# Lead-in of a fused attention and mixture kernel: keys and queries with neighbouring tokens in a partition, block means of the values as matrix products, loads in another order

## The chip, the core and the metric

The kernel runs on one NeuronCore of a Trainium2 chip. The core has TensorE for matrix products (it reads the on-chip memory SBUF and writes the accumulator memory PSUM, eight banks of 512 fp32 words in each of 128 partitions), VectorE and ScalarE for work on elements (both read and write PSUM and SBUF), GpSimd for constants, conversions and some DMA issues, and the sync engine SP, which issues most of the DMAs. Each engine works through its own queue of instructions in order; they meet in semaphores. A wait holds up everything behind it in that engine's queue. DMAs run on 16 DMA engines shared by all queues. The metric is the time of one execution on the device in microseconds (us).

## What is computed

Three stages follow each other. This case is about the first one only, and about its first half (the first of two batches).

```python
# q, k, v: (2, 8, 768, 64) fp32; block = 32, window = 16
k_sum = k.reshape(B, H, nb, block, D).max(axis=3)
v_sum = v.reshape(B, H, nb, block, D).mean(axis=3)      # 24 block means for each head
scores_l = scale * np.matmul(q, k.transpose(0, 1, 3, 2))
scores_s = scale * np.einsum('bhsd,bhnd->bhsn', q, k_sum) + np.log(block)
# scores_l outside |i - j| < 16 masked; softmax over both; then
out = np.matmul(a, np.concatenate([v, v_sum], axis=2))
# stage 2: dense mixture, sum over 4 experts of p_e * relu(x @ w1[e]) @ w2[e], x (1536, 512)
# stage 3: mixture of 8 experts with a skip score, one expert for each computed token
```

## The kernel before

**Tasks.** Attention is cut into 16 tasks `a`: two batches, two halves `s` of 384 queries, four pairs `n` of heads (`PAIRS`). One pair of heads fills 128 partitions (2 x 64). The keys of a pair are prepared once, for both halves of the batch: tasks 0 to 3 ("wide", `LEAD` = 4) prepare the keys of pairs 0 to 3. A task has six units of 64 queries; each unit sees a window of 96 keys and the 24 block maxima, `KW` = 120 columns.

**The path of a task.** SP loads keys (`load_keys`, L442) and queries (`load_queries`, L449) with tokens in partitions, one token of 64 numbers (256 bytes) in each run. TensorE transposes them into PSUM (`transpose_keys` L1750, six transposes of 128x128; `transpose_queries` L1760, three). ScalarE copies the windows of the keys (`copy_keys`, L850 to L852) and the queries (`copy_queries`, L858) to SBUF; VectorE takes the block maxima (`keys`, L1111 to L1116). TensorE forms the scores (`qk`, L1771, 24 products on tiles of 64x64). VectorE adds the mask and takes the negated maximum (`mask`, L1124, six), ScalarE takes exponentials in place (`exps`, L864, six), VectorE normalises (`norm`, L1132 to L1136, two). TensorE transposes the weights (`turn(a, h)`, L1785, three for each of two halves h), ScalarE evacuates them (`evac_t`, L870), TensorE multiplies with the values (`pv`, L1799, 24 products), ScalarE and VectorE split the result into a high and a low part (`high_o` L875, `low_o` L1142).

**Block means.** `v_all` holds for each unit 96 rows of values (`load_windows`) and 24 rows of block means. VectorE makes the means: `sum_values(c)` takes the values of four heads, 96 partitions with one block of 32 tokens each, halves them five times by additions (L1154: 1024, 512, 256, 128 and 64 columns) and scales (L1156). There are four such calls; c = 0 and 1 (first batch) stand on VectorE's queue ahead of `lead(0)` and `lead(1)`. GpSimd then spreads the means by DMA inside SBUF (`first_sums`, L732), two transfers for each task.

**Order in the lead-in.** It is written out by hand for each engine. On TensorE: keys, queries and scores of task 0, keys and queries of pair 1, and then `lead(a)` for a = 0, 1, 2: `spare` (14, 12 and 12 transposes of the identity, L1888, whose result nobody reads), `turn(a, 0)`, `qk(a + 1)`, `transpose_keys(a + 2)` while there are any, `transpose_queries(a + 2)`, `pv(a - 1)`, `turn(a, 1)`. Then `turn(3, 0)`, `pv(2)`, `turn(3, 1)`, `qk(4)`, `pv(3)`. From there on the first layer of stage 2 fills TensorE between the pieces of attention (L1845 to L1851 for the first block of features, then L1737 to L1739). In a lead ScalarE's order is `exps(a, 1)`, `copy_keys(a + 2)`, `copy_queries(a + 2)`, `exps(a + 1, 0)`, `evac_t(a, 0)`, `high_o(a - 1)`, `evac_t(a, 1)`; VectorE's is `mask(a + 1, 0)`, `norm(a, 1)`, `mask(a + 1, 1)`, `keys(a + 2)`, `norm(a + 1, 0)`, `low_o(a - 1)`. After the leads VectorE forms the low parts of the first layer's weights (`low_w1`, L1191, four pieces) with `low_o(2)` and `low_o(3)` between them. Their high parts are cast by GpSimd (`high_w1`, L737) from loads that GpSimd issues itself (`first_w1`, L723).

PSUM in the lead-in: banks 0 and 1 take transposed keys, 2 queries, 4 and 5 scores, 6 and 3 the two halves of `turn`, 7 the result of `pv`.

## Time and profile before

| | us |
|---|---|
| median of 3 runs | 728.18 |
| lowest, highest | 726.92, 729.25 |
| the profiled execution | 728.09 |
| its span, first to last instruction | 726.4 |

The profile shows one execution. Engines: PE is TensorE's products, PEld its loading of stationary operands, DVE is VectorE, ACT ScalarE, POOL GpSimd, SPq the queue of SP. A busy time of a group of pipelined instructions reaches to the end of the last one, so the next may start before it. The granted clock of TensorE (PEclk) is given as a share of 2.4 GHz; 0.5 is 1.2 GHz. Busy shares by engine over the span: PE 97%, PEld 80%, DVE 56%, ACT 39%, POOL 9%.

### The profile page before, as it was taken

How to read it: one execution, taken by the hardware profiler on the slowest of the kernel's cores; microseconds unless marked ns; L12 is line 12 of the kernel's file. 1: busy time of each engine (PE TensorE's matmuls, PEld its weight loads, DVE VectorE, ACT ScalarE, POOL GpSimd, SP SyncE). 2: the span in 40 equal slices, each digit the busy share in tenths (PEclk: the TensorE clock that was granted, in tenths of full speed). 3: DMA queues.
4: the chain of work that ended last, by engine and by line, in shares of the span. 5: the costliest groups of instructions: out<-in, count | busy, mean ns of one | idle time of the engine just before them, and what ended most of it. 6: DMA issues, size and time to landing. Idle time of an engine off the chain costs nothing.

```text
span 726.4 us, 12344 instructions
## 1 busy us (share of the span) xinstructions
PE 703.5 (97%) x4499; PEld 580.5 (80%) x4500; DVE 403.6 (56%) x1042; ACT 281.5 (39%) x653; POOL 66.2 (9%) x97
## 2 busy tenths in 40 slices
PE   5699999999999999999999999999999999999997
PEld 4588898898989889988988998899899884444444
DVE  4887674552895684754756364466447217453441
ACT  4745454451345534631621451064036112552430
POOL 2612000000000000000000000100000003232221
PEclk9989999999999999999999999999999999999999
DMA  9995632120709717713976739124530996799800
GB/s 205 216 209 107 134 82 64 32 48 12 279 17 335 322 51 291 284 63 103 418 301 278 261 116 363 53 107 179 226 116 3 373 361 232 288 394 393 332 2 22
DMA packets 92384, 139.36 MB, mean 192 GB/s; under 512 B 55172, under 2 KB 55456, under 8 KB 90656
## 3 DMA queue, kind: packets, MB, share of 16 engines
q1 hardware_dynamic: 89664, 133.89, 53.4%
q0 software_dynamic: 2656, 4.66, 2.0%
q8 instruction: 35, 0.57, 0.3%
q14 instruction: 29, 0.24, 0.1%
HBM read 104.05 MB, written 34.98 MB: 191 GB/s over the span
## 4 chain that ended last, share of the span: by engine, by line
PE 92%; DVE 5%; ACT 1%; issue 1%; DMA 0%; POOL 0%; SPq 0%; POOLq 0%; DVEq 0%; ACTq 0%
PE ps L1737 15%; PE ps L1739 15%; PE ps L1738 15%; PE ps L1987 8%; PE ps L1989 8%; PE ps L1988 8%; PE ps L2126 7%; PE ps L2098 7%; PE ps L1799 2%; PE ps L1771 2%; PE ps L1785 1%; PE ps L1930 1%; PE ps L2111 1%; PE ps L1750 1%; DVE acc L1154 1%
## 5 line engine op out<-in xcount | busy, mean ns | idle before, releaser
L1987 PE MATMUL ps<-xt_hi,wb_hi 128*128 128x384 f32 x336 | 112.8, 336 | 0.0
L1989 PE MATMUL ps<-xt_hi,wb_lo 128*128 128x384 f32 x336 | 112.4, 334 | 0.0
L1988 PE MATMUL ps<-xt_lo,wb_hi 128*128 128x384 f32 x336 | 112.3, 334 | 0.0
L969 ACT ACTIVATE h_raw<-ps 128x384 f32<-128x384 f32 x96 | 47.1, 490 | 116.1 <-PE ps L1989 114.0
L1738 PE MATMUL ps<-v_lo_acc,hb_hi 128*128 128x512 f32 x216 | 84.2, 390 | 0.0
L1363 DVE SCALAR_TENSOR_TENSOR acc<-ps,dp,acc 128x512 f32<-128x512 f32 x36 | 27.0, 750 | 99.3 <-PE ps L1739 99.3
L1348 DVE TENSOR_TENSOR h_raw<-ps,h_raw 128x384 f32<-128x384 f32 x96 | 49.7, 552 | 44.4 <-PE ps L1989 44.3
L975 ACT ACTIVATE hb_hi<-h_raw 128x384 fp32r<-128x384 f32 x96 | 49.0, 525 | 52.5 <-DVE h_raw L1348 52.5
L1987 PEld LDWEIGHTS ps<-xt_hi,wb_hi 128*128 128x128 f32 x336 | 63.1, 188 | 0.4
L1988 PEld LDWEIGHTS ps<-xt_lo,wb_hi 128*128 128x128 f32 x336 | 63.1, 188 | 0.3
L1989 PEld LDWEIGHTS ps<-xt_hi,wb_lo 128*128 128x128 f32 x336 | 63.1, 188 | 0.0
L1353 DVE SCALAR_TENSOR_TENSOR hb_lo<-h_raw,hb_hi 128x384 fp32r<-128x384 f32 x96 | 50.6, 554 | 14.6 <-ACT hb_hi L975 14.4
L1737 PE MATMUL ps<-v_hi_first,hb_hi 128*128 128x512 f32 x144 | 56.8, 395 | 0.0
L1739 PE MATMUL ps<-v_hi_first,hb_lo 128*128 128x512 f32 x144 | 56.2, 390 | 0.0
L2098 PE MATMUL ps<-sets,under 128*64 128x512 f32 x224 | 52.9, 611 | 0.2 <-DVE under L1551 0.2
L2126 PE MATMUL ps<-sets,acc 128*64 128x256 f32 x448 | 51.6, 382 | 0.7 <-ACT acc L1044 0.7
L783 POOL DMA_INDIRECT route_list<-entry,slot x12 | 12.1, 1010 | 402.2 <-DVE slot L1502 399.5
L1738 PEld LDWEIGHTS ps<-v_lo_acc,hb_hi 128*128 128x128 f32 x216 | 40.5, 188 | 8.1
L2126 PEld LDWEIGHTS ps<-sets,acc 128*64 128x64 f32 x448 | 31.4, 137 | 17.7 <-issue 3.2
L1737 PE MATMUL ps<-xt_hi,w_hi 128*128 128x384 f32 x124 | 43.9, 354 | 0.3 <-DVE h_lo L1200 0.3
L1739 PE MATMUL ps<-v_hi_next,hb_lo 128*128 128x512 f32 x108 | 42.1, 390 | 0.0
L1737 PE MATMUL ps<-v_hi_next,hb_hi 128*128 128x512 f32 x108 | 42.0, 389 | 0.0
(268 smaller groups left out, 1299.9 us busy)
## 6 DMA issues: line engine op xcount, KB each, us to landing
sets<-in_moe_w SPq DMA_DIRECT2D x72, 512.0 KB
w_aside<-wb_hi SPq DMA_DIRECT2D x3, 3584.0 KB, 17.0
w_aside<-wb_lo SPq DMA_DIRECT2D x3, 3584.0 KB, 24.7
wb_hi<-w_aside SPq DMA_DIRECT2D x21, 512.0 KB, 10.7
wb_lo<-w_aside SPq DMA_DIRECT2D x21, 512.0 KB, 11.5
acc<-in_moe_w SPq DMA_DIRECT2D x12, 768.0 KB, 5.2
w_raw<-in_moe_w SPq DMA_DIRECT2D x12, 512.0 KB, 5.6
stage<-in_k SPq DMA_DIRECT2D x16, 192.0 KB, 4.5
```

Source lines behind the costliest of these rows:

```text
L969: nc.scalar.activation(h_raw[:, f, half * GT:(half + 1) * GT], ps[:, bank, 0:GT], ACT.Copy).then_inc(put_by, 1)
L975: nc.scalar.activation(hb_hi[cols], h_raw[cols], ACT.Relu).then_inc(hb_hi_ok, 1)
L1348: TT(to, ps[:, bank, 0:GT], to, ALU.add).then_inc(joined, 1)
L1353: nc.vector.scalar_tensor_tensor(out=hb_lo[cols], in0=h_raw[cols], scalar=0.0, in1=hb_hi[cols].bitcast(F32), op0=ALU.max, op1=ALU.subtract ...
L1737: mm(dst, a_hi, b_hi, start=start, stop=False)
L1738: mm(dst, a_hi, b_lo, start=False, stop=False)
L1739: return mm(dst, a_lo, b_hi, start=False, stop=stop)
L1987: mm(to, wb_hi[w], hi(c), start=(c == 0 and not onto), stop=False, skip_group_check=onto)
L1988: mm(to, wb_hi[w], lo(c), start=False, stop=False, skip_group_check=onto)
L1989: last = mm(to, wb_lo[w], hi(c), start=False, stop=(c == HALF_D - 1), skip_group_check=onto)
L2098: last = mm(ps[j * QT:(j + 1) * QT, 0, 0:FQ], of[:, from_c:from_c + QT], wset[:, 0, at:at + FQ], start=(c == 0), stop=(c == KC - 1))
L2126: last = mm(ps[j * QT:(j + 1) * QT, bank, 0:DQ], ht2[:, at:at + QT], wset[:, 0, to:to + DQ], start=(f == 0), stop=(f == FC - 1))
```

## The change

Four things are changed, all for the first batch:

1. Keys are loaded with two neighbouring tokens in a partition (`KRUN` = 2, runs of 512 bytes), queries of tasks 0 to 4 with three (768 bytes). Each token set is then turned by one product with the identity for each head, on half of the columns of TensorE, and the result is written with a step of two or three words, so that the tokens stand in order. Six transposes for the keys of a pair become twelve products, three for the queries six.
2. The block means of the first batch come from TensorE. Values are loaded with six neighbouring tokens in a partition (`load_early`, four transfers of 192 KB); `in_block` holds 1/32 where a token is in a block and 0 elsewhere. `block_means(c)` is six products of 128x32 stationary and 256 moving columns that add up in bank 3. ScalarE copies the result (`copy_means`), and `first_sums` spreads it in one transfer instead of two. `turn(a, 1)` for a < 2 waits for that copy. VectorE's `sum_values(0)` and `sum_values(1)` go.
3. SP's loads: early values behind the queries of task 1, windows and second values behind the keys and queries that are due before them. GpSimd issues two loads of w1 ahead of `first_sums(1)`, and they no longer wait for the sums.
4. On TensorE `pv(3)` comes ahead of `qk(4)`.

```diff
+    KRUN = 2
+        early_k = [r.rearrange("p t h d -> p (t h d)").rearrange("p (h c t d) -> p h c t d", h=2, c=TP // KRUN, t=KRUN) for r in raw_k]
+        early_q = [r.rearrange("p t h d -> p (t h d)").rearrange("p (h t d) -> p h t d", h=2, t=TH) for r in raw_q]
+        SPAN = S // P
+        NBP = 32
+        v_early = h_raw[:, 2:6, :].rearrange("p f (j c) -> p (f j) c", j=2)
+        in_block = under_v2_hi[:, 0, 0:SPAN * NBP].rearrange("p (t n) -> p t n", t=SPAN)
+        means = h_rows[0:2 * NBP, UH * KW:UH * KW + 4 * DH]
...
 (load_keys)
-                    sp.dma_start(raw_k[m % 2][:, :, h, :], kh[2 * m + h].rearrange("(t p) d -> p t d", p=P)).then_inc(k_in[m % 2], 16)
+                    if m < PAIRS:
+                        sp.dma_start(early_k[m % 2][:, h, :, :, :].rearrange("p c t d -> p c (t d)"),
+                                     kh[2 * m + h].rearrange("(c p t) d -> p c (t d)", p=P, t=KRUN)).then_inc(k_in[m % 2], 16)
...
+            def load_early(c):
+                for h in range(4 * c, 4 * c + 4):
+                    sp.dma_start(v_early[:, h, :], vh[h].rearrange("(p t) d -> p (t d)", p=P)).then_inc(v_in[c], 16)
...
             load_queries(1)
-            load_values(0)
-            load_windows(0)
+            load_early(0)
             load_keys(2)
             load_queries(2)
-            load_windows(1)
-            load_values(1)
+            load_windows(0)
             load_keys(3)
             load_queries(3)
+            load_early(1)
+            load_windows(1)
             load_queries(4)
...
 (GpSimd)
+            nc.gpsimd.memset(in_block[:, :, :], 1.0 / BLOCK).then_inc(s_const, 1)
+            (two affine_select on in_block)
             def first_w1(c):
-                if c:
-                    gp.wait_ge(vsum_ok, 2)
             def first_sums(a):
-                gp.wait_ge(vsum_ok, n // 2 + 1)
+                gp.wait_ge(means_ok, n // 2 + 1)
...
             first_sums(0)
-            first_sums(1)
             first_w1(0)
             first_w1(1)
+            first_sums(1)
             first_w1(2)
             first_w1(3)
...
 (ScalarE, lead)
                 exps(a + 1, 0)
+                if a < 2:
+                    copy_means(a)
                 evac_t(a, 0)
...
+            def copy_means(c):
+                rows = slice(NBP * c, NBP * c + NB)
+                act.wait_ge(means_ps, c + 1)
+                nc.scalar.activation(means[rows, :], ps[rows, 3, 0:4 * DH], ACT.Copy).then_inc(means_ok, 1)
...
 (VectorE)
             norm(0, 0)
-            sum_values(0)
             lead(0)
-            sum_values(1)
             lead(1)
...
 (TensorE, transpose_keys; transpose_queries likewise with a step of TH = 3)
+                    if m < PAIRS:
+                        at += t // KRUN * KRUN * P
+                        for h in range(2):
+                            last = mm(ps_flat[h * DH:(h + 1) * DH, at + t % KRUN:at + KRUN * P:KRUN], early_k[m % 2][:, h, t // KRUN, t % KRUN, :], ident[:, :],
+                                      start=True, stop=True)
...
 (turn)
+                if a < 2 and h == 1:
+                    pe.wait_ge(means_ok, a + 1)
...
+            def block_means(c):
+                if c == 0:
+                    pe.wait_ge(s_const, 16)
+                else:
+                    pe.wait_ge(pt_ready, 2)
+                pe.wait_ge(v_in[c], 16 * 4)
+                for t in range(SPAN):
+                    last = mm(ps[NBP * c:NBP * (c + 1), 3, 0:4 * DH], in_block[:, t, :], v_early[:, 4 * c:4 * c + 4, t * DH:(t + 1) * DH],
+                              start=(t == 0), stop=(t == SPAN - 1))
+                last.then_inc(means_ps, 1)
...
 (lead)
                 if a + 2 <= LEAD:
                     transpose_queries(a + 2)
+                if a < 2:
+                    block_means(a)
                 if a:
                     pv(a - 1)
                 turn(a, 1)
...
             turn(LEAD - 1, 1)
+            pv(LEAD - 1)
             qk(LEAD)
-            pv(LEAD - 1)
```

## Rows read from the trace of the kernel before

**Rows 1.** The page: engines over the span, and the ended chain by engine.
```profile
PE 703.5 (97%) x4499; PEld 580.5 (80%) x4500; DVE 403.6 (56%) x1042; ACT 281.5 (39%) x653; POOL 66.2 (9%) x97
...
PE 92%; DVE 5%; ACT 1%; issue 1%; DMA 0%; POOL 0%; SPq 0%; POOLq 0%; DVEq 0%; ACTq 0%
```

**Rows 2.** Windows: stretch, length, busy by engine (instructions), granted clock, DMA share, GB/s.
```profile
0.00:48.20 48.20, 32.62 (x374) 27.47 (x375) 33.87 (x128) 25.53 (x93) 17.77 (x38) 0.93 0.95 210
48.20:716.00 667.80, 665.37 (x4080) 549.45 (x4081) 368.52 (x911) 255.36 (x559) 46.48 (x57) 1.00 0.54 193
...
36.80:43.40 6.60, 6.30 (x61) 5.54 (x62) 6.06 (x10) 1.77 (x5) 0.11 (x1) 0.52 0.75 164
```

**Rows 3.** Chain of waits of the lead-in: start, length, what held it.
```profile
1.31 3.06 DMA stage<-in_k
...
15.28 1.14 DVE acc L1154
...
22.60 1.22 DVE acc L1154
```

**Rows 4.** Timeline of TensorE: start, busy, line, result and operands, count, idle before.
```profile
4.50 1.52 PE L1750 MATMUL ps<-ident,stage 128*128 128x128 f32 x6 [4.50 <-DMA stage<-in_k]
...
15.33 0.54 PE L1785 MATMUL ps<-ident,h_rows 128*120 128x128 f32 x3 [1.33 <-DVE h_rows L1136]
...
16.58 0.87 PE L1750 MATMUL ps<-ident,stage 128*128 128x128 f32 x6
17.29 0.49 PE L1760 MATMUL ps<-ident,stage 128*128 128x128 f32 x3
19.91 0.54 PE L1785 MATMUL ps<-ident,h_rows 128*120 128x128 f32 x3 [2.12 <-DVE h_rows L1136]
20.29 1.47 PE L1888 MATMUL ps<-ident 128*128 128x128 f32 x12
22.74 0.54 PE L1785 MATMUL ps<-ident,stage 128*120 128x128 f32 x3 [0.98 <-DVE stage L1136]
...
25.15 0.92 PE L1799 MATMUL ps<-stage,v_first 120*64 120x64 f32 x24
...
30.22 0.54 PE L1785 MATMUL ps<-ident,h_rows 128*120 128x128 f32 x3 [1.03 <-DVE h_rows L1136]
...
37.10 0.90 PE L1785 MATMUL ps<-ident,stage 128*120 128x128 f32 x3 [0.44 <-DVE stage L1136]
```

**Rows 5.** Timeline of ScalarE in the first two leads.
```profile
17.49 0.25 ACT L850 ACTIVATE k_low<-ps 128x96 f32<-128x96 f32 x1 [1.90 <-PE ps L1750]
...
18.91 0.42 ACT L864 ACTIVATE stage<-stage,nmax 128x120 f32<-128x120 f32 x1
...
20.05 0.93 ACT L870 ACTIVATE stage<-ps 120x384 f32<-120x384 f32 x2
...
26.32 0.41 ACT L864 ACTIVATE h_rows<-h_rows,nmax 128x120 f32<-128x120 f32 x1
```

**Rows 6.** Timeline of VectorE behind the leads, and where TensorE's unbroken stretch begins.
```profile
36.96 1.22 DVE L1191 TENSOR_TENSOR w_lo<-acc,w_hi 128x1024 fp32r<-128x1024 f32 x1
...
41.45 0.56 DVE L1142 TENSOR_TENSOR xt_lo<-ps,xt_hi 128x384 fp32r<-128x384 f32 x1 [0.54 <-ACT xt_hi L875]
41.92 1.22 DVE L1191 TENSOR_TENSOR w_lo<-acc,w_hi 128x1024 fp32r<-128x1024 f32 x1
...
48.23 0.44 PE L1737 MATMUL ps<-xt_hi,w_hi 128*128 128x384 f32 x1
```

**Rows 7.** Chain of waits of the third stage: fp32 products on tiles of 128x64.
```profile
640.36 3.60 PE ps L2126 x32
```

**Rows 8.** DMA: packets of 12 to 15 and 30 to 33 us; one issue, 0 to 70.
```profile
DMA packets 2578, 0.64 MB, mean 213 GB/s; under 512 B 2578, under 2 KB 2578, under 8 KB 2578
...
DMA packets 789, 1.00 MB, mean 332 GB/s; under 512 B 579, under 2 KB 579, under 8 KB 788
...
v_first<-stage POOLq DMA_DIRECT2D x4, 36.0 KB, 5.3
```

More of the change, by code:

```diff
@@ L1146, in sum_values @@
             def sum_values(c):
[L1147 to L1148 removed]
+                rows, k = v_rows, c - 2
+                dve.wait_ge(v_in[k], 16 * 4 + 16)
                 left = BLOCK * DH
```

77 lines of the change are left out of this document (49 added, 28 removed).

## Prediction

> **What bounds the kernel now.** I read the page's engine line and chain first. TensorE is busy 97% of the span and is 92% of the chain that ended last [rows 1]. The table by stretches then says where its idle time lies. From 48.2 us to 716 us it is busy 665.37 of 667.80 us, but before 48.2 us only 32.62 of 48.20 [rows 2]. The change touches the attention of the first eight head pairs, so what counts is by how much the unbroken stretch of TensorE, which starts with the matmul at 48.23 [rows 6], can start earlier; everything behind it slides along. The profiled execution took 728.09 us (span 726.4 and 1.7 around it) and the median of the three runs is 728.18, so the sum is made on either.
>
> Inside the lead-in I read the chain of waits. It runs over the load of the first keys and then over VectorE: the five halving additions of the values (L1154) stand in it twice, from 15.28 and from 22.60 [rows 3]. With the four smaller additions and the scaling each of the two sums takes about 3.15 us. The reader who stops here would credit the change with 6.3 us. The decisive step is the next one: for each lead, what else had to be waited for, had VectorE been free? For this I lay TensorE's and ScalarE's rows of the same stretch side by side [rows 4, 5].
>
> **The leads without the sums.** lead(0) lasts from the transposes of turn(0,0) at 15.33 to those of turn(1,0) at 22.74, 7.41 us; lead(1) from 22.74 to 30.22, 7.48 us [rows 4]. Count from the start of each:
> - The key transposes begin at +1.25 (16.58 in lead(0)), and ScalarE's copies of them start at +2.16 (17.49).
> - ScalarE works in a fixed order: three key copies, the query copy, then the exponentials of the next task. They begin at +3.58 in both leads (18.91; 26.32) and end at +4.72, where today the next copy starts (20.05) [rows 5]. In lead(0) these rows follow each other without a gap, so VectorE isn't what makes them late: with the sums gone its masks are ready sooner, and ScalarE still gets there at +3.58.
> - The change puts `copy_means` behind these exponentials, and lets turn(a,1) on TensorE wait for it, since both use PSUM bank 3. No row has a copy of 24 partitions x 256; the copy of 128x96 takes 0.25 us and one 120x384 about 0.46 (0.93 for two) [rows 5], which bounds it by 0.25 and 0.46. I take 0.36, between them by its columns, and 0.1 for the hand-over. So turn(a,1) starts at +5.2. In lead(0) it is at +4.58 today (19.91) [rows 4]: the new wait makes it 0.6 later, not earlier. Queued behind it on TensorE are the fill transposes and turn(a+1,0); behind `copy_means` on ScalarE stand both evacuations.
> - Then come turn(a,1), 0.38 us up to the fill transposes (19.91 to 20.29), and the twelve fills of `spare`, 1.47 busy (20.29) or about 1.42 until the next can start [rows 4]. Today VectorE's wait hides them; now they are on the path. 5.2 + 0.38 + 1.42 = 7.0 us per lead.
>
> So a lead goes from 7.41 and 7.48 to 7.0: 0.4 + 0.5 = **0.9 us** saved where the row of VectorE promised 6.3. lead(2) has no sum and no means; turn(2,0) at 30.22 to turn(3,1) at 37.10 [rows 4] stays as it is.
>
> **Keys and queries by products.** Six key transposes become twelve fp32 products of 128x64 stationary and 128 moving columns. The nearest row is L2126, the same 128x64 tiles in pairs with 256 columns: 32 in 3.60 us, 112 ns each [rows 7]. Half the columns make 56 to 61 ns, twelve 0.67 to 0.73 us; six transposes take 0.71 (16.58 to 17.29) [rows 4]. I count them at nothing, and the queries (six for three) too. What rows can't show is a result with a step of two or three words in PSUM. Bounds: from the rate that 64x64 tiles reach, which would save 0.3 us a time, to no pairing at all, 118 ns each, twice as long.
>
> The Trainium skill speaks against this edit: "TensorEngine Tiling (Array Packing)", Restrictions and Gotchas, says that column tiling excludes the transpose mode for fp32 input, and "TensorE: Matmul & The Clock Gate", Terms, that this mode is four times faster for FP32. The row of L2126 disagrees on the size of it; its result is a rival below.
>
> **The first load.** The chain starts with 3.06 us of the first keys, up to 4.37 [rows 3]. 384 KB in runs of 256 B move at 213 GB/s, in a stretch with mostly large runs at 332 [rows 8]: 1.8 against 1.2 us. Runs of 512 B lie between; the second of the two loads still has to be issued after the first. Bounds 0 and 0.6, taken: **0.3 us**.
>
> "DMA: Bandwidth & Descriptors", Why small descriptors are slow, in the Trainium skill gives 3 cycles on top of 8 for 256 B; as an estimate 384 KB would then need 14% less, 0.25 us, which is near what I take.
>
> **Loads in another order.** Queries end at +2.3 in a lead (17.29 plus 0.35) [rows 4], so `block_means` asks for its values at about 17.3 and, with lead(1) starting at 22.0, at 24.3. The first 768 KB are issued from 5.2 us on and land by 10 at 213 GB/s. The second are issued by SP behind the waits for the second keys' and queries' transposes (12 us) and behind four transfers of keys and queries; even at 213 GB/s [rows 8] for the 1.4 MB of these and themselves they land near 20. I count nothing; if they are late, TensorE stands in front of pv(0) and turn(1,1). GpSimd's loads of w1 no longer wait for VectorE's second sum; VectorE starts on w1 at 36.96 with no idle time before it [rows 6], so having its high part earlier is worth nothing, and the loads only share the queues with the second values. `first_sums(0)` is issued at about 20.3, and its transfer takes 5.3 us at the median to land [rows 8]; pv(0) wants it at 25.6 (24.3 and 1.35 for the means). Just in time, counted as nothing; 1 us late would still be before turn(1,1).
>
> **block_means.** Six products of 256 columns onto one group of 32 columns, so none can run beside another. Bounds: 112 ns each, as in pairs, 0.67 us; four times the columns' time unpaired, 2.7. Taken: twice the pair's 112, 1.35 us, since a pair takes 225. In lead(0) TensorE is idle 2.12 us before turn(0,1) [rows 4], and in lead(1) pv(0) behind it (0.92 busy) [rows 4] ends at +4.6, against the +5.2 of turn(1,1): covered; at 2.7 us it would cost 0.7. The tile `in_block` costs GpSimd three more instructions before 8.5 us, while TensorE asks at 17.
>
> **The end of the lead-in.** After turn(3,1) VectorE runs without a pause from 36.96 to the last low part of w1 (41.92, 1.22 long), but for 0.54 us in which it waits at 41.45 for ScalarE's copy behind pv(3) [rows 6]. The change puts pv(3) ahead of qk(4). It then waits for low_o(2), which is behind the first low part, so it starts near +1.7 after turn(3,1) rather than +2.2, and the 0.54 us go: **0.5 us**. Next on VectorE's queue are the masks and normalisations of task 4, which bring the matmul at 48.23; they shift by as much. The clock of 1.2 GHz in 36.80:43.40 (mean 0.52) [rows 2] costs TensorE there, but VectorE's chain is the longer, so I give nothing for it.
>
> **Sum.** 0.3 + 0.4 + 0.5 + 0.5 = 1.7 us: 728.09 - 1.7 = **726.4**, from the median 728.18 also about 726.4. With the bounds of the parts: 725.4 to 727.4.
>
> **The rivals.**
> - *Products cheaper than transposes* (lower bound above): 0.3 us in each of two leads, half in the third, twice that in two early stages at 1.2 GHz, where the six take 1.52 instead of 0.87 us [rows 4]: up to 2.2 more. About 725.0. Chance 0.15.
> - *The full credit*: VectorE's 6.3 us come off, 721.8. For it: the chain [rows 3]. Against it: ScalarE's gapless rows [rows 5]. 0.04.
> - *The clock falls inside the leads.* TensorE's filling gets thinner: `block_means` uses a quarter of the columns, and then TensorE stands 1.5 us for `copy_means`. If the grant goes to 1.2 GHz there, for as long as the 6.6 us seen at the end [rows 2], the path from turn(0,1) to the key products (0.38 + 1.42 + 1.25 + 0.71 = 3.8 us) doubles: 726.4 + 3.8 = **730.2**. Before the change the same stretch kept 2.4 GHz with a pause of 2.1 us; but it had VectorE as its bound, so that a fall cost little. Chance 0.16, half of it beyond +0.3%.
> - *No pairing*: every product takes a transpose's 118 ns. Keys +0.7 in two leads, queries +0.35 in the third, +1.3 twice in the stages at 1.2 GHz: +4.4, **730.8**, slower. Over 82 ns a product the kernel is slower than before, near 111 by more than 0.3%. 0.09.
> - *Four times*: a pair at 4 x 118 ns gives +2.1, +2.1, +1.05 and twice +4.2, 740.0. That is what the skill's two sentences amount to. 0.03.
> - *It doesn't do what it says*: values late, or the keys land no earlier, 727.5. 0.07.
> - My forecast: 0.46.
>
> **Chances.** Within 0.3% means 726.0 to 730.4, about what can be told from no change. Faster: 0.14 of the forecast's 0.46 lies under 726.0, with 0.15 and 0.04 that is 0.33. Slower: 0.08 + 0.09 + 0.03 = 0.20. Same 0.47. For 8 in 10 the range leaves out the full credit, the four times, part of the unpaired case and of the cheap products: 724.2 to 730.5.
>
> **What would show it.** Right: in the profile after, turn(0,1) starts on ScalarE's copy of the means and not on VectorE, the fill transposes run straight into turn(1,0), leads of 7.0 us, VectorE with idle time in the leads, and the unbroken stretch from about 46.5. A key step of 0.7 us at 2.4 GHz shows the products right, 1.4 wrong. A granted clock under 1 between 16 and 34 us shows the third rival. If the leads measure near 4.5 us, my reading of ScalarE's order is wrong.

## The result: slower, and where the time went

The kernel after took 731.43 us (median of 13 runs, 729.42 to 735.36) against 728.18 for the kernel before (13 runs, 726.54 to 730.49): a ratio of 1.0051, 95% interval 1.0036 to 1.0065. It is slower by half a per cent where the forecast was 1.8 us faster, and it lies above the range. The profiled execution of after took 732.84 us, with a span of 731.1: 1.4 us above its kernel's median, while that of before lies on its own.

The page of the kernel after; its lines answer to [rows 1]: the span, the engines over it, and the ended chain by engine.
```profile
span 731.1 us, 12622 instructions
...
PE 714.1 (98%) x4640; PEld 589.7 (81%) x4641; DVE 400.4 (55%) x1030; ACT 282.3 (39%) x655; POOL 64.3 (9%) x96
...
PE 95%; DVE 2%; issue 1%; ACT 1%; DMA 0%; POOL 0%; SPq 0%; POOLq 0%; ACTq 0%
```
TensorE is busy 10.6 us more, with 141 instructions more, and VectorE's share of the chain has gone from 5% to 2%. VectorE was indeed taken off the path; TensorE has taken its place and more.

Stretches of the kernel after, as in [rows 2] (stretch, length, busy by engine, granted clock, DMA share, GB/s).
```profile
0.00:54.60 54.60, 44.76 (x514) 37.15 (x516) 29.53 (x116) 26.59 (x95) 16.43 (x37) 0.91 0.70 189
54.60:721.00 666.40, 663.98 (x4084) 549.08 (x4084) 369.60 (x911) 255.09 (x559) 45.92 (x57) 1.00 0.54 193
40.40:50.60 10.20, 9.45 (x91) 8.16 (x92) 9.09 (x26) 4.20 (x17) 1.04 (x1) 0.52 0.67 157
```
The unbroken stretch of TensorE begins at 54.67 us instead of 48.23, 6.4 later; TensorE's busy time ahead of it is 12.1 us more, with 140 more instructions. What follows is the same work: from there to the end it is 678.2 us before and 676.4 after. Those 1.7 us are a second stretch of the lower clock, at 610.1 to 613.5 us of the profiled run of before, that this run of after doesn't have; of the twelve profiled runs below seven have one between 609 and 632 us (those without fills but with products, without sums, with the casts in a row, with the other order at the end, both with the means in the fills' place and GpSimd's casts, and with half the heads by transposes) and five don't. It comes and goes with edits that don't touch that stage, so it isn't put down to the change. So the loss stands wholly in the lead-in.

TensorE in the kernel after (start, busy, line, result and operands, count, idle before), against [rows 4].
```profile
4.26 2.83 PE L1789 MATMUL ps<-ident,stage 128*64 128x128 f32 x24 [4.26 <-DMA stage<-in_k]
6.84 1.52 PE L1805 MATMUL ps<-ident,stage 128*64 128x128 f32 x12
...
11.29 2.83 PE L1789 MATMUL ps<-ident,stage 128*64 128x128 f32 x24
...
17.69 0.55 PE L1834 MATMUL ps<-ident,h_rows 128*120 128x128 f32 x3 [0.28 <-DVE h_rows L1174]
...
18.94 1.53 PE L1789 MATMUL ps<-ident,stage 128*64 128x128 f32 x24
20.30 0.83 PE L1805 MATMUL ps<-ident,stage 128*64 128x128 f32 x12
21.05 2.78 PE L1859 MATMUL ps<-h_raw,under_v_hi 128*32 128x256 f32 x12
24.39 0.52 PE L1834 MATMUL ps<-ident,h_rows 128*120 128x128 f32 x3 [0.55 <-ACT h_rows L951]
24.74 1.47 PE L1950 MATMUL ps<-ident 128*128 128x128 f32 x12
26.05 0.49 PE L1834 MATMUL ps<-ident,stage 128*120 128x128 f32 x3
...
29.36 2.78 PE L1859 MATMUL ps<-h_raw,under_v_hi 128*32 128x256 f32 x12
...
34.61 0.49 PE L1834 MATMUL ps<-ident,h_rows 128*120 128x128 f32 x3
...
40.58 0.89 PE L1834 MATMUL ps<-ident,stage 128*120 128x128 f32 x3 [2.08 <-DVE stage L1174]
...
42.88 0.90 PE L1834 MATMUL ps<-ident,stage 128*120 128x128 f32 x3
```
The counts (the last number, x24 and the like) are what to look at. `transpose_keys` issues twelve products for a pair and the row has x24; `transpose_queries` issues six, x12; `block_means` six, x12. A product of plain fp32 is recorded as two matmul instructions, a transpose as one (the fills, x12 for twelve). A pair of keys takes 1.36 us from start to start (18.94 to 20.30), where the six transposes took 0.71; the means take 2.72. There is no idle time between turn(0,0) at 17.69 and the end of the means.

The chain of waits from the end of `qk(1)` to `turn(1,0)`, against [rows 3]: no VectorE in it.
```profile
19.01 1.46 PE ps L1789 x24
20.47 0.66 PE ps L1805 x12
21.12 2.72 PE ps L1859 x12
23.87 0.38 ACT h_rows L951
...
24.39 0.52 PE ps L1834 x3
24.90 1.31 PE ps L1950 x12
```

From turn to turn the 6.4 us split so, each from the starts in the two timelines:

| stretch | before | after | difference |
|---|---|---|---|
| start to turn(0,0) | 15.33 | 17.69 | +2.36 |
| lead(0): turn(0,0) to turn(1,0) | 7.41 | 8.36 | +0.95 |
| lead(1): turn(1,0) to turn(2,0) | 7.48 | 8.56 | +1.08 |
| turn(2,0) to turn(3,1) | 6.88 | 8.27 | +1.39 |
| turn(3,1) to the long stretch | 11.13 | 11.79 | +0.66 |

The second and third are longer products: the run with transposes below, which differs by them and their loads alone, has leads of 7.38 and 7.57. The first holds longer products too, but also how long TensorE works at half its rate at the start, which differs between profiled executions of the same instructions (see the run without fills). In all, 6.4 us in one pair of profiled executions is more than the 3.25 us between the medians. The fourth has a cause of its own, seen when VectorE and GpSimd are laid side by side (kernel after, timelines of the two engines):
```profile
36.54 0.58 DVE L1170 TENSOR_SCALAR rsum<-rsum 128x3 f32<-128x3 f32 x1
37.15 0.18 DVE L1172 RECIPROCAL rinv<-rsum 128x3 f32<-128x3 f32 x1
...
38.42 1.32 DVE L1170 TENSOR_SCALAR rsum<-rsum 128x3 f32<-128x3 f32 x1
39.77 0.18 DVE L1172 RECIPROCAL rinv<-rsum 128x3 f32<-128x3 f32 x1
...
38.66 1.05 POOL L768 CAST w_hi<-acc 128x1024 fp32r<-128x1024 f32 x1
```
An addition on 128x3 values, 0.17 us elsewhere, takes 1.32 and ends 0.03 us behind GpSimd's cast of a piece of w1. turn(3,0) waits for it. The one at 36.54 lost 0.41 us in the same way, to a cast from 36.05 to 37.09. The kernel before has the same effect, but smaller, 0.20 and 0.14 us (its VectorE, beside casts from 33.00 and 35.18):
```profile
33.70 0.37 DVE L1132 TENSOR_SCALAR rsum<-rsum 128x3 f32<-128x3 f32 x1
...
35.95 0.31 DVE L1132 TENSOR_SCALAR rsum<-rsum 128x3 f32<-128x3 f32 x1 [0.64 <-ACT stage L864]
```
In the fifth stretch TensorE is granted 0.52 of its clock (1.2 instead of 2.4 GHz) for 10.2 us, from 40.4 to 50.6, where it was 6.8 us before, from 36.7; the lower level begins while TensorE stands idle ahead of turn(3,0), as the row at 40.58 shows. This accounts for the whole +0.66. From turn(3,1) to the long stretch TensorE is busy 11.06 of 11.13 us before and 11.21 of 11.79 after, at a mean granted clock of 0.73 and 0.69; length times clock is 8.1 us in both, and 8.1 to 8.2 in five of the kernels below; the others have more waits in this stretch, and 8.4 to 9.8.

### The profile page after: what moved, and what is told of

Read it like the earlier page. It is cut to its first block, busy times and chain, and to the rows that moved or that the text cites. A ratio compares the mean times of both kernels' runs of the same rounds, so it can differ in the third digit from the quotient of the medians.

```text
span 731.1 us, 12622 instructions
## 1 busy us (share of the span) xinstructions
PE 714.1 (98%) x4640; PEld 589.7 (81%) x4641; DVE 400.4 (55%) x1030; ACT 282.3 (39%) x655; POOL 64.3 (9%) x96
## 4 chain that ended last, share of the span: by engine, by line
PE 95%; DVE 2%; issue 1%; ACT 1%; DMA 0%; POOL 0%; SPq 0%; POOLq 0%; ACTq 0%
PE ps L1773 15%; PE ps L1775 15%; PE ps L1774 15%; PE ps L2049 8%; PE ps L2051 8%; PE ps L2050 8%; PE ps L2188 7%; PE ps L2160 6%; PE ps L1848 2%; PE ps L1818 2%; PE ps L1834 2%; PE ps L1789 1%; PE ps L1992 1%; PE ps L2173 1%; PE ps L1859 1%
## 5 line engine op out<-in xcount | busy, mean ns | idle before, releaser
L1389 DVE SCALAR_TENSOR_TENSOR hb_lo<-h_raw,hb_hi 128x384 fp32r<-128x384 f32 x96 | 50.6, 555 | 14.6 <-ACT hb_hi L1013 14.4
L814 POOL DMA_INDIRECT route_list<-entry,slot x12 | 12.1, 1007 | 402.2 <-DVE slot L1538 399.4
```

The lines of the kernel that those rows point to most:

```text
L1389: nc.vector.scalar_tensor_tensor(out=hb_lo[cols], in0=h_raw[cols], scalar=0.0, in1=hb_hi[cols].bitcast(F32), op0=ALU.max, op1=ALU.subtract ...
```

## The experiments

Each ratio is to the kernel before as timed in the same session, where its median was 727.05 to 727.85 us. Times within the lead-in are from one profiled execution of each kernel. "The long stretch" is the start of the unbroken stretch of TensorE, 48.23 before and 54.67 after. Three theories stood at first: (1) products are two instructions and take twice what I gave them, on a path that is now TensorE's; (2) the block means and the fills made the loss; (3) it is only the longer stretch at 1.2 GHz.

**Each half alone.** The kernel before with products and wide loads for keys and queries, sums still on VectorE:
```diff
 (kernel before; load_keys and load_queries as in the change, and in transpose_keys, queries likewise)
+                    if m < PAIRS:
+                        at += t // KRUN * KRUN * P
+                        for h in range(2):
+                            last = mm(ps_flat[h * DH:(h + 1) * DH, at + t % KRUN:at + KRUN * P:KRUN], early_k[m % 2][:, h, ...], ident[:, :], ...)
```


> The kernel before with nothing changed but the loads and the turning of keys and queries: runs of 512 and 768 bytes, products with the identity instead of transposes; sums of the values on VectorE, order of the loads and of pv(3) and qk(4) as before. Theory 1 (an fp32 product runs as two instructions and costs what two transposes cost): keys 1.36 us instead of 0.71 at 2.4 GHz and 2.6 instead of 1.3 in the two early stages at 1.2 GHz, so turn(0,0) comes 1.7 to 2.4 us later than at 15.33, and the unbroken stretch 1.6 to 3 us later than at 48.23: 729.8 to 731. In the leads VectorE's sums still hide most of it. Theory 2 (the loss of the change lies in the block means and in the fills, and the products are about as dear as transposes): 727.9 to 728.5. Theory 3 (the loss is only a longer stretch at 1.2 GHz at the end of the lead-in): no change in the leads, 728 to 730 as the clock falls.

728.85 us, ratio 1.0023 (1.0006 to 1.0039), which is 729.9 on the 728.18 that the forecast started from; the long stretch from 49.57. turn(0,0) is 2.0 us later and the leads as long as before (7.40 and 7.47), as theory 1 had it. The long stretch came only 1.3 us later, not 1.6 to 3, since the granted clock didn't fall behind turn(3,1) in this execution (mean 1.00). And the kernel after with keys and queries loaded and transposed as before:
```diff
-    for h in range(2):
-        last = mm(ps_flat[h * DH:(h + 1) * DH, at + t % KRUN:at + KRUN * P:KRUN], early_k[...], ident[:, :], ...)
+    last = nc.tensor.transpose(ps_flat[:, at:at + P], raw_k[m % 2][:, t, :, :]..., ident[:, :])
```


> The changed kernel with keys and queries loaded and transposed as before; block means on TensorE, order of the loads, pv(3) ahead of qk(4) as changed. Theory 1: the leads begin at 15.4 as before; block_means takes 2.7 us and pushes ScalarE's copy, so turn(0,1) at 21.0 instead of 19.91, turn(1,0) at 22.8, turn(2,0) at 30.4, as before the change: 728.2 to 728.9, no gain and little loss. Theory 2 (means and fills are the loss): 731 or more. Theory 3 (clock): 729 to 731 with a stretch at 1.2 GHz longer than 7 us.

728.89 us, ratio 1.0014 (0.9995 to 1.0033); the long stretch from 49.18. Alone the two halves put it off by 1.3 and 0.9 us, together by 6.4. For the leads the reason is in [rows 4]: before the change TensorE idles 2.1 and 1.0 us ahead of its turns in a lead, behind VectorE, so longer products hide there, and the means' price of 2.72 us leaves the leads at 7.38 and 7.57 with transposes. Once the sums are off VectorE nothing is left to hide longer products: from the second kernel to the kernel after, which differ by the products and loads alone, the two leads grow by 0.98 and 0.99 us. That is 2.0 of the 4.2 us by which the whole is more than the sum of the halves. The other 2.4 stand behind turn(3,1), where the clock was higher in both halves (mean 1.00 and 0.77, against 0.69), and -0.3 between. The long stretch moves by 5.5 us from the second kernel to the kernel after, of which 2.05 stand ahead of turn(0,0). In medians, which were taken in two sessions, it is less: 1.0014 to 1.0051 of the kernel before. The medians don't show that the whole is more than the sum: 0.23% and 0.14% against 0.51%, each known to some 0.15%.

**The fills.** The kernel after without the 24 fill transposes that ran on the path:
```diff
-    SPARE = (14, 12, 12)
+    SPARE = (14, 0, 0)
```


> The changed kernel without the fill transposes of lead(1) and lead(2) (24 of 38). If the fills stand on the path, as the trace of after shows (1.31 us each in the chain), turn(1,0) and turn(2,0) come 1.3 and 2.6 us earlier than in the changed kernel and the time falls by 1.3 to 2.6 us, to 729 to 730. If the clock theory holds, a thinner TensorE loses 2.4 GHz earlier and longer and the time doesn't fall or rises, 731.5 to 734.

729.55 us, ratio 1.0020 (1.0003 to 1.0037); the long stretch from 50.86, 3.8 us sooner than in the kernel after. But 2.0 of the 3.8 stand ahead of turn(0,0), where no instruction differs (kernel after without fills, TensorE):
```profile
10.60 1.53 PE L1789 MATMUL ps<-ident,stage 128*64 128x128 f32 x24
...
15.71 0.54 PE L1834 MATMUL ps<-ident,h_rows 128*120 128x128 f32 x3 [1.24 <-DVE h_rows L1174]
```
The second pair's twelve products take 1.36 us up to the queries here (10.60 to 11.96) and 2.61 in the kernel after (11.29 to 13.90), though the column of the granted clock reads 1.00 from 4 us on in both. TensorE goes from half to full rate at about 9.8 us here, at 12 to 13 before, and behind 15.3 in the profiled execution of after. So the +2.36 of the table is not the products' price alone: with an early rise the same instructions cost +0.38. The fills themselves are worth 1.30 us in lead(0) and 0.85 in lead(1), 2.15 together, which is what the medians show (1.0051 to 1.0020, 2.3 us).

turn(2,0) is at 30.48, nearly back at 30.22. Most of the rest of the way to 48.23 is lost in lead(2), 8.71 us long against 6.88 before, where TensorE waits 0.82 us for sums ahead of pv(1), 1.54 for VectorE ahead of turn(3,0) and 0.35 for sums ahead of pv(2). This chain of waits shows where the last comes from:
```profile
26.74 4.48 issue
31.24 0.98 POOL w_hi L768
32.22 5.24 DMA v_first<-h_rows
```
pv(2) waits for the sums of task 2 ("batch" in the expectations below is a task too). Their load stands in GpSimd's queue behind the first cast of w1, and GpSimd had stood idle 4.5 us ahead of the cast, for the load of w1.

**The sums' price, by leaving them out.** The kernel before with only the scaling of the first two sums left:
```diff
+                    if c < 2:
+                        dve.sem_inc(vsum_step, 1)
+                        continue
```


> The kernel before with the five halving additions left out for the two sums of the first batch (the scaling stays, so the block means of the first batch are wrong). It measures alone what VectorE's sums cost the kernel. Forecast's step (ScalarE's order holds the leads): turn(0,1) at 18.2, turn(1,0) at 21.1, turn(2,0) at 26.8, a gain of 2.5 to 3.5 us, 725 to 725.7, of the 5.9 us taken away. Full credit: 722.2. If the leads don't depend on VectorE at all: 728.

Its total, 738.17 us (ratio 1.0143), can't be read as a price, since wrong means change the data of the later stages, and so probably the routing of tokens in the third. Its lead-in can: turn(0,0) to turn(1,0) is 5.87 us instead of 7.41, so of the 2.9 us of additions taken away (15.28 to 18.20 in the chain of before; the scaling stays) 1.5 come off, and turn(0,1) comes at 18.34 instead of 19.91. In lead(1) the gain ends at a load (kernel before without sums, TensorE):
```profile
23.00 0.87 PE L1753 MATMUL ps<-ident,stage 128*128 128x128 f32 x6 [0.45 <-DMA stage<-in_k]
27.14 0.91 PE L1763 MATMUL ps<-ident,raw_q 128*128 128x128 f32 x3 [3.26 <-DMA raw_q<-in_q]
```
What held the path next was the load of the queries, issued at 17.0 behind the windows and 10.1 us under way, with a load of w1 issued at 18.95 beside it.

**Means by products, no fills, transposes kept.** The kernel after, with both edits:
```diff
 (keys and queries loaded and transposed as before, and)
+    SPARE = (14, 0, 0)
```


> The changed kernel with keys and queries transposed and loaded as before the change, and no fills at turn(1,0) and turn(2,0), so that of the three edits the block means by products stand alone with fewer fills about them. Theory (each product is two instructions, a step too many on the path costs its whole length): block_means stands on the path with 2.75 us in lead(0) and lead(1), ahead of turn(a,1); the 26 fills that went were worth 1.5 + 1.3 us of TensorE's order. turn(1,0) at about 21.7, turn(2,0) at about 28.5, the long stretch of TensorE from about 48.0 against 48.23 before: 727.0 us, -0.4 against the kernel before. Rival A (the fills only filled waits): as the kernel with old transposes and all fills, 728.9. Rival B (the wait for the load of the queries or for batch 2's sums, which stand in GpSimd's queue behind a cast, takes their place, as in the run of the changed kernel without fills, where pv(2) waited 5.2 us for them): the long stretch from 50 or later, 729 or more.

725.42 us (8 runs, 724.33 to 726.78), ratio 0.9969 (0.9955 to 0.9983), the long stretch from 46.57: faster than before, and 1.6 us under what was expected (turn(2,0) came at 28.51 as expected, what follows was 1.4 us shorter). It differs from the kernel with transposes above by the fills alone: ratio 1.0014 to 0.9969, long stretch 2.6 us sooner. It differs from the kernel with no fills above by the products and wide loads alone: that one has a ratio of 1.0020, leads longer by 0.97 and 0.86 us from nearly the same turn(0,0) (15.57 and 15.71), and a long stretch 4.3 us later. The control has the sums on VectorE:
```diff
 (kernel before)
-    SPARE = (14, 12, 12)
+    SPARE = (14, 0, 0)
```


> The kernel before with one edit alone: no fills at turn(1,0) and turn(2,0), as in the run with transposes and without fills that came out at 725.42, so that the two differ by the block means (and the order of loads and of pv(3)) alone. Theory (with the sums on VectorE the leads are bound by VectorE and ScalarE, and the fills lie in TensorE's wait for them): leads as before, 7.4 and 7.5 us, the long stretch from 48.2, total 727.4; then the block means by products are worth 0.3% once no fills stand about them. Rival (the fills themselves cost the kernel before 1.5 us, and the block means nothing): the long stretch from 46.7, total 725.6. A third way (without fills TensorE's clock falls within the leads): 728.5 or more.

728.59 us, ratio 1.0003 (0.9988 to 1.0019); turn(2,0) at 30.43 against 30.22 before, the long stretch from 48.88. The theory holds: with the sums on VectorE the fills are free; the block means by products, with the other order of the loads and of pv(3), are worth about 0.3% once no fills stand on the path with them. The third way of the expectation was seen too: without fills the granted clock is 0.50 from 23.0 to 26.5 us in lead(1), behind idle times of 2.12 and 2.29 us. It cost little, since VectorE bounds that lead.

**What makes a product dear.** The kernel after, with the first head's half turned by transposes on the same operands and into the same strided places:
```diff
+    if h == 0:
+        nc.tensor.transpose(ps_flat[0:DH, at + t % KRUN:at + KRUN * P:KRUN], early_k[m % 2][:, 0, ...], ident[:, :])
+        continue
```


> The changed kernel with the first head's half of the keys and queries turned by transposes that read and write what the products did (the same 64-column operand, the same strided output on partitions 0 to 63), and the second head's half by products as before; block means untouched. Theory (a product of plain fp32 runs as two instructions, a transpose as one): twelve operations of a pair of keys are recorded as 6 + 12 = 18 instructions, six of a query batch as 3 + 6 = 9, and a pair of keys takes 18 x 57 ns = 1.02 us at the full clock instead of 1.36, a query batch 0.51 instead of 0.68. On the path in lead(0) and lead(1): -0.5 us each, and -0.5 or so ahead of the first scores; the long stretch from 53.2 instead of 54.67, total 730.0. Rival (the strided write or the 64-column shape is what costs, whatever the kind of instruction): the six transposes are recorded as twelve or take 113 ns each, times as those of the changed kernel, 731.4.

750.4 us (5 runs), ratio 1.0295, the long stretch from 66.41. The counts came out as the theory said (this kernel, TensorE, in lead(0)); the times did not.
```profile
24.33 0.30 PE L1790 MATMUL ps<-ident,stage 128*64 128x128 f32 x1
24.56 0.43 PE L1792 MATMUL ps<-ident,stage 128*64 128x128 f32 x2
24.92 0.30 PE L1790 MATMUL ps<-ident,stage 128*64 128x128 f32 x1
25.15 0.43 PE L1792 MATMUL ps<-ident,stage 128*64 128x128 f32 x2
```
The transposes are x1 and the products x2, each on the same 128x64 tile: it is the kind of operation, not its shape or its stride, that makes two instructions. But a transpose and a product together take 0.59 us from start to start (24.33 to 24.92) at 2.4 GHz, where two products in a row take 0.23 (1.36 us for twelve). So the 1.02 us expected for a pair of keys was 3.56. Two things changed with the edit: the halves of a pair of heads no longer follow each other as products on the two halves of the columns, and TensorE goes from one kind to the other at each step. What each of them costs is bounded by the means, which are alone on their columns and take 2.72 us for six of 256, so 0.23 us for 128. A lone product of 0.23 and a transpose of at most 0.12 make 0.35, and 0.24 us are left for the two changes of kind, 0.12 each: an estimate, which no run here takes apart. Nor does any run have transposes of 64 columns by themselves, so part of the 0.24 may be their own price.

So the price list is this: 128 columns of a lone fp32 product take 0.23 us, of two on the two halves of the columns 0.11 each, of a transpose 0.12 for twice the stationary columns. That the two heads' products run beside each other is read from this half price; no run has them one at a time. The Trainium skill ("FP8 and Floating Point Precision", TensorE Precision Notes) says that true fp32 makes four passes through the array; 128 columns at 2.4 GHz four times are 0.21 us, an estimate, and the trace agrees with 0.23. The Trainium skill ("TensorE: Matmul & The Clock Gate", Terms) calls the transpose mode four times faster for FP32; the measured 0.12 against a lone product's 0.23 is twice, and the measurement decides.

**GpSimd's casts.** The kernel with transposes and no fills, with GpSimd's queue in another order:
```diff
-            high_w1(0)
             first_sums(2)
-            high_w1(1)
-            high_w1(2)
+            for c in range(PIECES):
+                high_w1(c)
             first_sums(3)
-            high_w1(3)
```


> As the run with transposes and without fills, but GpSimd issues the sums of the first values for batch 2 ahead of its first cast of w1, then does the four casts in a row and issues those of batch 3 last. Theory (a small operation of VectorE in lead(2) takes 1.3 us instead of 0.16 while GpSimd casts, and pv(2) waits for sums that stand behind a cast): the casts lie from about 32 to 37 us, VectorE's slow operation moves or goes, the wait at pv(2) goes; the long stretch starts 1 us or more before that of the kernel without this order, about 47.5: 726.5 us. Rival (the casts slow whatever VectorE does beside them, wherever they stand, so that only the place moves): within 0.3 us of that kernel. Second rival (the sums for batch 3 come too late now): pv(3) waits, 0.5 to 1 us later.

726.93 us, ratio 0.9996 (0.9983 to 1.0010), long stretch from 47.58, 1.0 later than without the order. The first rival had the mechanism right, though not the size: the stall moved to another place, where it costs more (this kernel, VectorE, then GpSimd):
```profile
29.62 0.28 DVE L1152 CUSTOM_DVE_ANT_0 stage<-ps,neg_mask 128x120 f32<-128x120 f32 x1 [0.52 <-PE ps L1797]
...
30.24 1.65 DVE L1160 TENSOR_SCALAR rsum<-rsum 128x3 f32<-128x3 f32 x1
...
28.85 3.00 POOL L760 CAST w_hi<-acc 128x1024 fp32r<-128x1024 f32 x3
```
The addition on SBUF waits until the casts end at 31.85; the mask at 29.62, which reads PSUM, takes its usual 0.28 us in the midst of them.

**The order at the end.** The kernel before, with pv(3) ahead of qk(4):
```diff
+            pv(LEAD - 1)
             qk(LEAD)
-            pv(LEAD - 1)
```


> The kernel before with one edit alone: pv(3) stands ahead of qk(4) at the end of the lead-in, as in the changed kernel. Theory of the prediction: the wait at pv(3) is filled less, the first step of the following part is reached up to 0.5 us sooner: 726.9 us. Rival (the order of the two doesn't matter, since the same work stands between turn(3,1) and the long stretch): no change, 727.4. Rival from the other side (qk(4) had filled the wait of pv(3) for its softmax): 0.5 to 0.9 us later, 728.1.

728.84 us, ratio 1.0012 (1.0000 to 1.0023). pv(3) starts 1.48 us after turn(3,1) instead of 2.23, as forecast, but the long stretch follows turn(3,1) by 11.28 us instead of 11.13. The 0.5 us of the forecast don't come: at mean clocks of 0.72 and 0.73, length times clock is 8.1 us in both, so the order is worth nothing. It is TensorE, busy 11.06 of these 11.13 us, that bounds the stretch before, and not VectorE; at a clock of 1.00, in the kernel before with products, TensorE does have idle time there, and the stretch is 9.83 us. Its turn(3,1) itself is 0.94 later than before, though the edit comes after it: in the chain of waits VectorE took 0.87 us for the small addition at 32.51, beside a cast from 32.30, and in its timeline 1.20 instead of 0.53 for the normalisation at 35.14, beside one from 34.90. This is the size by which the casts' timing moves a profiled execution.

**The means placed in the fills' place.** The kernel after, with keys and queries transposed, the loads in the order of use and the casts in a row; block_means(0) ahead of turn(0,0), where the 14 fills stood, block_means(1) into bank 7 after turn(0,1). The main lines:
```diff
-    SPARE = (14, 12, 12)
+    SPARE = (0, 0, 12)
 (lead)
-                if a < 2:
-                    block_means(a)
...
                 turn(a, 1)
+                if a == 0:
+                    block_means(1)
...
+            block_means(0)
             for a in range(LEAD - 1):
 (GpSimd)
+            gp.wait_ge(tq_done, 4)
             first_w1(0)
```


> The block means by products, placed where they don't stand ahead of a turn: those of batch 0 take the place of the 14 fills ahead of turn(1,0), those of batch 1 go into a bank of their own after turn(0,1) in place of the 12 fills; keys and queries by transposes from loads of the old form, which go out in the order of use; the casts of w1 in a row ahead of batch 3's sums. Theory (a product is two instructions; the three adds of VectorE were 3.2 us of the old leads, of which 1.5 were on the path; 2.75 us of products in the place of 1.5 us of fills cost 1.2 at most): leads of about 5.9, 6.0 and 6.5 us instead of 7.4, 7.5 and 6.9, turn(2,0) at about 27.5, turn(3,1) at about 34.5, the long stretch from about 45.5 against 48.23 before: 725 us, -2.5 or so. Rival A (loads become the bound once the leads are shorter, as in the run without sums, where turn(1,1) waited for the queries until 27): the long stretch from 48 or later, 727.5. Rival B (a shorter lead-in lets TensorE's clock fall later in it, by 1 us or more of lost time): 726.

729.32 us, ratio 1.0014 (1.0000 to 1.0027), the long stretch from 50.10. The leads came nearly as forecast: turn(0,0) at 16.37, 1.0 us later than before, since the means stand ahead of it (the 14 fills stood there, and not ahead of turn(1,0), as the expectation has it); then 6.18 us to turn(1,0) and 5.88 to turn(2,0) at 28.43. Then Rival A: the loads of w1, from 25.3 on, the windows of task 2 beside them, and task 3's sums behind the casts; pv(2) at 36.59, pv(3) at 40.01. With w1 loaded earlier:
```diff
-            gp.wait_ge(tq_done, 4)
+            gp.wait_ge(tq_done, 3)
```


> The kernel with the block means in the place of fills, with one edit: GpSimd issues w1's loads once the third batch of queries is turned instead of the fourth, about 19 us instead of 25.3, in the stretch from 21 to 26.5 us in which the DMA engines stood idle. Theory (that run lost its gain to w1's loads and batch 2's windows sharing the DMA, the casts behind them and batch 3's sums behind the casts: pv(2) waited until 36.6, pv(3) until 40.0): the casts lie from 27 to 32, pv(2) starts at about 33.5, pv(3) at about 36.5, the long stretch from about 45.5 against 50.1: 724.8 us. Rival A (the windows of batch 2 alone bound pv(2) whatever shares the DMA: they are issued after pv(0) and took 5.7 us in the run without fills): the long stretch from 46.5, 725.7. Rival B (w1's loads now delay what the third and fourth pair of keys wait for, ahead of 26 us): leads longer, 728.

730.02 us, ratio 1.0022 (1.0008 to 1.0036), against a forecast of 724.8. The loads were no longer late, but now all four casts ran in a row in lead(1) (this kernel, VectorE, GpSimd, TensorE):
```profile
26.80 4.10 DVE L1145 COPY k_low<-k_sum 128x144 f32<-128x144 f32 x1
30.82 0.22 DVE L1146 COPY k_high<-k_sum 128x144 f32<-128x144 f32 x1
...
26.82 3.98 POOL L760 CAST w_hi<-acc 128x1024 fp32r<-128x1024 f32 x4
...
31.95 0.90 PE L1815 MATMUL ps<-ident,h_rows 128*120 128x128 f32 x3 [4.45 <-DVE h_rows L1166]
```
A copy of 0.23 us takes 4.1 and ends 0.1 us after the fourth cast; TensorE idles 4.45 us behind it, and behind that idle time the clock granted from 31.9 to 38 us is 0.50, the lower level: the three transposes of a turn take 0.90 us instead of 0.54. One edit more tests this cause: ScalarE does the casts, behind its exponentials of task 3.
```diff
 (GpSimd)
-            for c in range(PIECES):
-                high_w1(c)
 (ScalarE)
             exps(LEAD - 1, 1)
+            cast_w1(0)
             high_o(LEAD - 2)
             evac_t(LEAD - 1, 0)
             evac_t(LEAD - 1, 1)
+            cast_w1(1)
+            cast_w1(2)
+            cast_w1(3)
```


> The run before this one (means in the place of fills, w1 loaded at 19 us), with one edit: the four casts of w1 that GpSimd did are done by ScalarE, one behind the last exponentials of batch 3 and three behind its last copy. In that run VectorE's copy of 144 keys (L1145, 0.23 us elsewhere) took 4.02 us, from 26.88 to 30.90, and GpSimd's four casts ran from 26.82 to 30.80. Theory (an operation of VectorE waits out a cast of GpSimd that runs beside it): with the casts gone from GpSimd that copy takes 0.23 us again, turn(2,0) starts at about 28.2 instead of 31.95, pv(2) at about 33.4, pv(3) at about 36, the long stretch at about 45.5 instead of 50.8: 724.5 us. Rival (something else held VectorE there, the loads of 512 KB that fill the DMA or the order of its queue): the copy still takes 4 us and turn(2,0) stays at 32. Second rival (ScalarE's casts, 1.1 us each, now hold up its copies and the products of the first w1 step): the copy is short but the long stretch starts at 47 or later, 726.5.

725.36 us (12 runs, 724.41 to 727.35), ratio 0.9976 (0.9963 to 0.9990). The same rows of this kernel:
```profile
26.41 0.23 DVE L1147 COPY k_low<-k_sum 128x144 f32<-128x144 f32 x1
...
27.69 0.54 PE L1817 MATMUL ps<-ident,h_rows 128*120 128x128 f32 x3 [0.57 <-DVE h_rows L1168]
...
45.33 0.42 PE L1767 MATMUL ps<-xt_hi,w_hi 128*128 128x384 f32 x1
...
48.89 0.92 PE L1831 MATMUL ps<-stage,v_first 120*64 120x64 f32 x24 [1.21 <-DMA v_first<-h_rows]
```
The copy is back at 0.23 us, and turn(2,0) and the long stretch are at 27.69 and 45.33, where 28.2 and 45.5 were forecast. The last row accounts for the difference between 2.9 us less of lead-in and some 1.7 us in the median: task 4's sums, loaded behind the shorter lead-in, are now late by 1.2 us. This kernel and the one with transposes and no fills are equal within what was measured, both faster than before and after.

## Why the prediction was wrong, step by step

- **Keys and queries by products, counted at nothing: the step that failed.** It took the x32 of [rows 7] for 32 products of 112 ns. They are 16, of 225 ns, each recorded twice. A pair of keys costs 1.36 us and not 0.71, and queries 0.75 and not the 0.35 to 0.41 of three transposes: 0.98 and 0.99 us in the two leads against the run with transposes, 0.23 in lead(2), and 1.3 for each of the two pairs of keys turned at half rate ahead of turn(0,0) (the load gave 0.24 of it back, which leaves the +2.36; where the rate rises early it is less, +0.38 in the run without fills). The rival at 118 ns a product, 730.8 us, had the right size (113) for a wrong reason: the products do pair, but at twice the price taken. The trace of before could have told: `qk` and `pv` issue twelve products each, not the 24 that the section on the kernel gives, and stand in every timeline as x24.
- **block_means: mis-sized by the same count.** Taken 1.35 us, bounds 0.67 to 2.7; measured 2.72, the upper bound. It was to be covered; with the keys later too it ended at +6.15 from the lead's start. ScalarE, to be ready at +4.72, was itself late by the keys and ready at +5.5 (23.18); so the means cost 0.7 us beyond the keys, as the text had put it for this bound. With transposes kept, this price alone leaves the leads at 7.38 and 7.57 us where 7.0 was forecast, and with it the gain of 0.9 us is gone.
- **ScalarE's order and copy_means: right.** turn(a,1) starts on ScalarE's copy (24.39, released by it), and the copy took 0.37 us against 0.36. It came at +6.70 instead of +5.2, all of it the two points above.
- **Fills on the path: right**, with 0.35 and 1.31 us for 0.38 and 1.42 in the forecast. So the leads were 8.36 and 8.56 instead of 7.0, and lie where the steps put them once the two prices are corrected: 7.0 + 1.5 - 0.14 = 8.36.
- **The first load: right.** TensorE starts at 4.26 instead of 4.50, 0.24 us for 0.3. Over all the profiles it starts at 4.20 to 4.42 in the four kernels with wide loads and at 4.50 to 4.87 in the others.
- **Loads in another order: right at nothing.** No wait on values or w1 is in the chain of after; from first_sums(0), issued at 25.0, nothing waits.
- **The end of the lead-in: wrong.** -0.5 was forecast, and it was +0.66 with the change and +0.15 alone. pv(3) did come sooner, but nothing behind it did. The step took VectorE's chain for the longer one; TensorE, at 1.2 GHz for 6.0 us of the stretch, was busy for all but 0.07 us of it. The longer time at 1.2 GHz, 7.3 us of the stretch for 6.0, is the difference: half of 1.3 is 0.65.
- **Not foreseen: GpSimd's casts.** 1.15 and 0.41 us in lead(2), against 0.14 and 0.20 in the kernel before. Their place beside VectorE's small operations is a matter of tenths of a microsecond, which every change of the lead-in moves.
- **The clock.** It did not fall inside the leads, as the third rival had it; the transposes of a turn take 0.49 to 0.55 us up to and with that at 37.95. It fell longer after them. In other kernels it did fall in a lead, without fills as told above, and in the one with the other order at the end from 20.4 to 23.9 us, behind the same 2.12 us of idle time that left it at 2.4 GHz before; VectorE's sums, on the path there, hid it. So the forecast's comfort from the kernel before, that a pause of 2.1 us kept 2.4 GHz, was one execution's.
- **A sum.** The terms named for the cheap products add up to 1.95 us, not 2.2; nothing hangs on it.

The direction was lost with one misread count, used for two prices: the means' price takes the gain (1.0014 with transposes), and the products' makes the loss (1.0051 with them; without fills 0.9969 and 1.0020). Of the 6.4 us of the profiled executions 4.4 stand ahead of turn(2,0), where the products' price, and for about 2 us the moment at which TensorE's rate rises, differ from the forecast; 1.4 are in lead(2), the cast above all, and 0.7 behind it, the clock.

## What to carry to other kernels

Divide a row's time by the number of operations in the code, not by the count in the trace: an fp32 product is two instructions there, and costs twice what a transpose of the same data costs even when two heads share the array. Moving work from a busy engine to an idle one also takes away the idle time in which that engine's other steps, fills among them, were free, so price each of them again as if it stood alone on the path. Before moving a step in time, look at what GpSimd does on SBUF beside it. And compare two profiled executions stretch by stretch, from a point up to which the kernels are the same: the first 15 us of one kernel can differ by 2 us from those of another with the same instructions.

## What the runs showed of the hardware

- Plain fp32 products: 0.23 us for 128 columns alone at 2.4 GHz (means, 21.05), 0.11 each for two 64-column tiles in turn (keys, 18.94), two recorded instructions per product. Transposes of fp32: 0.12, one instruction.
- Alternating transposes with lone fp32 products costs 0.59 us a pair at 2.4 GHz and 0.97 at half rate (4.57 to 5.54 in the same kernel), against 0.35 for the two at 2.4 GHz. What of it is the change of kind is not shown.
- In the first microseconds the column of the granted clock reads 1.00 while rows take twice as long as later (twelve products 2.61 us against 1.36), up to 9.8 us in one profiled execution and beyond 15 in another of the same instructions.
- From turn(3,1) to the long stretch, length times mean granted clock is 8.1 to 8.2 us in seven kernels, with lengths of 10.59 to 11.79.
- Operations of VectorE with operands in SBUF alone waited out GpSimd's casts: 1.32 us for 0.17 in the kernel after, 1.65 beside three casts, 4.10 for 0.23 beside four, each ending within 0.1 us of the last cast. Masks that read PSUM ran at their usual 0.28 us meanwhile. The Trainium skill ("SBUF — State Buffer", Terms) tells of a port pair that VectorE and GpSimd lock against each other for a whole instruction; these rows agree, and add that a run of casts wasn't interrupted. By the recorded starts VectorE was first in two of them (38.42 against 38.66, 26.80 against 26.82) and waited all the same.
